# A hand-ordered attention pipeline: scores and kv products a chunk ahead, transposes two ahead, decay split over two engines, dummy products at the start

## What is computed

```
# 1. attention with a decaying state, per head (48 x 48 state)
for t in range(S):
    state = alpha[:, :, t, :, None] * state + einsum('bhd,bhe->bhde', k[t], v[t])
    y[:, :, t] = einsum('bhd,bhde->bhe', q[:, :, t], state)
# 2. Fourier mixing over tokens and width, then a normalised MLP
X = fft(fft(x, axis=1), axis=2);  u = x + real(X)
un = (u - mean(u)) / sqrt(var(u) + 1e-6);  x = u + relu(un @ w_ch1) @ w_ch2
# 3. a token MLP and a channel MLP
u = x + (relu(xT @ w_tok1) @ w_tok2)T;  out = u + relu(u @ w2_ch1) @ w2_ch2
```

## Time and profile before

| what | value |
|---|---|
| median of 3 runs | 998.97 us |
| the profiled execution | 999.33 us, span 997.5 us, mean granted clock 0.991 |
| PE matmuls busy | 926.2 us, 93% of the span |
| DVE, ACT, POOL busy | 473.4, 289.3, 246.7 us |
| chain that ended last | PE 63%, DVE 11%, issue 9%, POOL 6%, ACT 3% |
| stage 0, attention of sequence 0 | 9.07 to 84.5 us, PE busy 65.7 of 75.5 us |
| MLP of sequence 3, alone | 553 to 622 us, PE busy 68.9 of 69 us |
| third layer | 622 to 997 us, PE busy 369.4 of 375 us |

### The profile page before, as it was taken

One profiled execution on the slowest core, in us unless ns is written; L12 is line 12 of the kernel. 1 busy time (PEld: TensorE's weight loads), 2 busy tenths in 40 slices (PEclk: granted clock), 3 DMA queues, 4 the chain that ended last, 5 costly groups with the idle time before them and its releaser, 6 DMA issues.

```text
span 997.5 us, 14828 instructions
## 1 busy us (share of the span) xinstructions
PE 926.2 (93%) x5280; PEld 875.4 (88%) x5280; DVE 473.4 (47%) x1126; ACT 289.3 (29%) x746; POOL 246.7 (25%) x440
## 2 busy tenths in 40 slices
PE   5885689989999989999899999999999999999998
PEld 5774678879888879888799999899999999999998
DVE  5557676554865654865556321622142223313221
ACT  3552243323343332433332322322122112111111
POOL 3677134430244420344401142200020001002000
PEclk9999889999999999999999999999999999999999
DMA  9700402101222003022001600200010001000000
GB/s 280 258 1 1 107 1 54 54 25 44 64 77 56 1 25 107 25 54 55 1 25 46 220 36 1 107 13 24 24 47 0 24 24 47 24 0 24 0 24 24
DMA packets 14235, 50.48 MB, mean 51 GB/s; under 512 B 1392, under 2 KB 5616, under 8 KB 12240
## 3 DMA queue, kind: packets, MB, share of 16 engines
q1 hardware_dynamic: 13600, 46.60, 14.8%
q0 software_dynamic: 576, 3.15, 0.8%
HBM read 40.31 MB, written 9.44 MB: 50 GB/s over the span
## 4 chain that ended last, share of the span: by engine, by line
PE 63%; DVE 11%; issue 9%; POOL 6%; ACT 3%; DMA 0%; DVEq 0%; POOLq 0%; ACTq 0%; SPq 0%
PE bank L1154 20%; PE bank L1156 19%; PE bank L1155 19%; POOL dec L463 3%; DVE ext L714 2%; POOL qkap L447 1%; PE bank L1171 1%; DVE st L729 1%; POOL qkap L444 1%; ACT qz L537 1%; DVE xf L863 1%; DVE at L823 1%; PE bank L1184 1%; DVE tmp L828 1%; DVE hl L1012 1%
## 5 line engine op out<-in xcount | busy, mean ns | idle before, releaser
L1012 DVE SCALAR_TENSOR_TENSOR hl<-bank,hh 128x384 fp32r<-128x384 f32 x192 | 106.1, 552 | 307.6 <-ACT hh L627 307.6
L627 ACT ACTIVATE hh<-bank 128x384 fp32r<-128x384 f32 x192 | 94.0, 490 | 327.9 <-PE bank L1156 327.4
L463 POOL TENSOR_SCALAR dec<-st,suf 48x48 f32<-48x48 f32 x160 | 78.5, 491 | 144.1 <-DVE st L729 88.1
L1154 PE MATMUL bank<-w2h,hh 128*128 128x384 f32 x288 | 102.2, 355 | 5.7 <-DVE u L1027 5.6
L1154 PE MATMUL bank<-nh,w1h 128*128 128x384 f32 x288 | 103.7, 360 | 1.3 <-DVE nl L967 1.3
L537 ACT ACTIVATE qz<-qkap 48x128 f32<-48x128 f32 x192 | 59.2, 308 | 150.9 <-POOL qkap L447 141.2
L1154 PE MATMUL bank<-u2h,w3h 128*128 128x384 f32 x288 | 98.1, 341 | 0.8 <-DVE u2l L1110 0.8
L1156 PE MATMUL bank<-nh,w1l 128*128 128x384 f32 x288 | 98.4, 342 | 0.0
L1155 PE MATMUL bank<-nl,w1h 128*128 128x384 f32 x288 | 98.3, 341 | 0.0
L1154 PE MATMUL bank<-w4h,hh 128*128 128x384 f32 x288 | 97.9, 340 | 0.0
L1156 PE MATMUL bank<-u2h,w3l 128*128 128x384 f32 x288 | 97.5, 339 | 0.0
(11 more groups left out here) (138 smaller groups left out, 1858.2 us busy)
## 6 DMA issues: line engine op xcount, KB each, us to landing
qkap<-qka SPq DMA_DIRECT2D x15, 1008.0 KB, 6.4
vt<-v SPq DMA_DIRECT2D x16, 288.0 KB, 7.7
raw_a<-w_ch SPq DMA_DIRECT2D x6, 768.0 KB, 13.2
mid<-u SPq DMA_DIRECT2D x8, 576.0 KB, 2.7
raw_b<-w_ch SPq DMA_DIRECT2D x6, 768.0 KB, 5.8
xr<-mid SPq DMA_DIRECT2D x8, 576.0 KB, 4.1
out<-u SPq DMA_DIRECT2D x8, 576.0 KB, 2.7
raw_t<-w_tok SPq DMA_DIRECT2D x2, 768.0 KB, 5.1
```

The lines of the kernel that those rows point to most:

```text
L463: pool.tensor_scalar(dec[r, k % 2, e], st[r, (k - 1) % 3, e], suf[r, k % RING, 0:1], None, ALU.mult).then_inc(s_dec, 1)
L627: act.activation(hh[:, s % 4, :], bank[s % 2][:, 0:HALF], ACT.Relu).then_inc(s_hhi, 1)
L1012: dve.scalar_tensor_tensor(out=hl[:, s % 4, :], in0=bank[s % 2][:, 0:HALF], scalar=0.0, in1=hh[:, s % 4, :].bitcast(F32), op0=ALU.max, op1 ...
L1154: pe.matmul(out_ap, wh, rh, start=first, stop=False)
```

## The change

All four pieces of the visit are written anew.

- PE's visit k: scores and now the kv product of chunk k+1 (one semaphore for both), y and state product of chunk k, transpose of chunk k+2. The kv product moves from the y bank into the score bank, the transposed keys into the y bank. In sequences 1 to 3 PE waits at the front for `at` of k and `st` of k; stage 0 alternates two banks of each kind (4, 5 and 6, 7) and waits one visit further back.
- DVE's visit k: `at` of k+1, `st` of k+1 (it was k), scans of k+3. The two reductions of the range test move within the unit; in stage 0 the first unit's reductions read an extra copy of the decays (`alpha0`), and the first suffix product no longer stands behind them.
- POOL's visit k: the two scalings for k+3 first, then one half of `dec` for k+2. The other half is on ACT, at the end of its visit. `dec` gets a third buffer.
- ACT's visit k: `qz` of k+2, `krt` of k+2, `x` of k, its half of `dec` of k+2.
- A visit k = -2 is added in front: `PAUSES` loses slot 1. The scans of chunk 1 leave the Fourier tail of the sequence before and stand in visit -2.
- Stage 0: weight splitting on ACT every second visit from k = 6 (was every visit), on POOL every third from k = 9 (was every second from 10). SP issues queries and keys, then identity and mask, values, the copy of the decays, the other units, and last the flip matrix and column, which have a semaphore of their own. PE starts with 8 products of a zeroed tile, 384 columns each, before its first wait for data.

```diff
-PAUSES = (1, 3, 7, 14, 21, 28)
-VISIT = dict(zip([h for h in range(31) if h not in PAUSES], range(-1, STEPS)))
+PAUSES = (3, 7, 14, 21, 28)
+WARM = 8
+VISIT = dict(zip([h for h in range(31) if h not in PAUSES], range(-2, STEPS)))
...
+    def visit_bank(a, k):
+        return bank[6 + k % 2] if a == 0 else bank[7]
...
# POOL
-            def decay(a, k, lows=0):
...
+            def decay(a, k):
+                if 0 < k < STEPS and k % NC:
+                    pool.wait_ge(s_st, a * STATES + state_index(k - 1) + 1)
+                    pool.tensor_scalar(dec[0:D, k % 3, 0:D], st[0:D, (k - 1) % 3, 0:D], suf[0:D, k % RING, 0:1], None,
+                                       ALU.mult).then_inc(s_dec[0], 1)
+            def visit(a, k):
+                prep(a, k + 3)
+                decay(a, k + 2)
...
# ACT
                 for h in range(2):
                     attn_qz(a, k + 2, h)
-                attn_krt(a, k + 1)
+                attn_krt(a, k + 2)
                 if k >= 0:
                     attn_x(a, k)
+                decay(a, k + 2)
...
# DVE
-                if k >= 0:
-                    attn_state(a, k)
...
+                attn_state(a, k + 1)
+                prep(a, k + 3)
...
# PE
+            def visit(a, k):
...
+                was = k - (1 if a else 2)
+                if 0 <= k + 1 < STEPS:
+                    if was >= -1:
+                        pe.wait_ge(s_at, a * STEPS + was + 2)
+                    if has_state(was + 1):
+                        pe.wait_ge(s_st, a * STATES + state_index(was + 1) + 1)
+                    mm = attn_scores(a, k + 1)
+                    if has_state(k + 1):
+                        mm = attn_kv(a, k + 1)
+                    mm.then_inc(s_sc, 1)
...
+                if k >= 0:
+                    mm = attn_back(a, k)
+                if has_state(k + 2):
+                    mm = attn_turn(a, k + 2)
+                mm.then_inc(s_vis, 1)
...
+            pe.wait_ge(s_zero, 1)
+            for i in range(WARM):
+                pe.matmul(bank[0][:, 0:HALF], at[:, 0, 0, :], at[:, :, :, :].rearrange("p a h t -> p (a h t)")[:, 0:HALF],
+                          start=True, stop=True)
+            pe.wait_ge(s_const, 32)
```

More of the change, by code:

```diff
@@ L542, in attn_x, with decay @@
                     act.wait_ge(s_ua, a * UA)
-                act.wait_ge(s_y, a * STEPS + k + 1)
-                if k % NC < NC - 1:
-                    act.wait_ge(s_st, a * STATES + state_index(k) + 1)
-                act.activation(x[:, k % NC, (k // NC) * PW:(k // NC + 1) * PW], y_bank(a, k)[:, 0:PW], ACT.Copy
-                               ).then_inc(s_x, 1)
+                act.wait_ge(s_vis, visited(a, k))
+                act.activation(x[:, k % NC, (k // NC) * PW:(k // NC + 1) * PW], y_of(a, k), ACT.Copy).then_inc(s_x, 1)
+            def decay(a, k):
+                if 0 < k < STEPS and k % NC:
+                    act.wait_ge(s_st, a * STATES + state_index(k - 1) + 1)
+                    r = head_rows(1)
+                    act.activation(dec[r, k % 3, D:PW], st[r, (k - 1) % 3, D:PW], ACT.Copy, scale=suf[r, k % RING, 0:1]
+                                   ).then_inc(s_dec[1], 1)
             def visit(a, k):
@@ L619, in tail @@
                     norm_split(a, t)
-                if h == SLOTS - 1 and a + 1 < B:
-                    for half in range(2):
-                        attn_qz(a + 1, 0, half)
             def hidden(bi, s):
@@ L1006, in tail @@
                         extreme(a + 1, 0, i)
-                    for k in range(2):
-                        prep(a + 1, k)
+                    prep(a + 1, 0)
             def hidden(bi, s):
@@ L1186, in attn_back @@
                 if c:
-                    pe.wait_ge(s_dec, 2 * s)
-                    mm = pe.matmul(y[:, 0:PW], buf[0:PR, 0, cols], dec[0:PR, k % 2, :], start=False, stop=True)
-                mm.then_inc(s_y, 1)
-                if c < NC - 1:
-                    pe.wait_ge(s_krt, s + 1)
-                    pe.matmul(y[0:PR, KV_AT:KV_AT + PW], krt[:, s % 2, :], vb[:, c, :], start=True, stop=True
-                              ).then_inc(s_kv, 1)
+                    for h in range(2):
+                        pe.wait_ge(s_dec[h], a * STATES + state_index(k - 1) + 1)
+                    mm = pe.matmul(y, buf[0:PR, 0, cols], dec[0:PR, k % 3, :], start=False, stop=True)
+                return mm
+            def visit(a, k):
+                if k == -2 and a:
+                    pe.wait_ge(s_ua, a * UA)
+                    pe.wait_ge(s_nlo, (a - 1) * NC + 2)
+                was = k - (1 if a else 2)
+                if 0 <= k + 1 < STEPS:
+                    if was >= -1:
[6 more added lines that the diff above has]
+                    mm.then_inc(s_sc, 1)
+                if has_state(was + 2):
+                    pe.wait_ge(s_krt, a * STATES + state_index(was + 2) + 1)
+                if was >= 0:
+                    pe.wait_ge(s_x, a * STEPS + was + 1)
+                if k >= 0:
[3 more added lines that the diff above has]
+                mm.then_inc(s_vis, 1)
                 if k == FLAG - 1:
```

244 lines of the change are left out of this document (98 added, 146 removed).

## The result

| | median | runs | profiled execution | span |
|---|---|---|---|---|
| before | 998.97 us | 997.85 to 1000.9 (4) | 999.3 us | 997.5 us |
| after | 939.9 us | 938.46 to 943.73 (4) | 938.46 us | 936.7 us |

The ratio is 0.9413, with a 95% interval of 0.9381 to 0.9445: 59 us less, where 51 were forecast. The mean granted clock is printed as 0.991 before and 0.963 after; the first is too high, for it has 1.00 in stage 0, where score pairs took 1.09 us, against 0.61 at the higher level.

The account below looks back on a forecast made before the run. PE, busy 93% of the span, mostly with MLP matmuls, was taken as the bound. 999.3 - 39.3 (interleaved slots, clock) + 3.9 (sequence starts) - 16 (stage 0) = 947.9, forecast 948 us, own range 940 to 955, whole range 938 to 972.

Parts of the forecast that it names:

- The loop: Interleaved slots: a 3.87 us loop through POOL, ACT and DVE opens; 12.5 of 13.9 us of waits regained a sequence.
- The 1.2 us left for the reductions: Interleaved slots: PE waits of 1.2 us a sequence, expected to remain because of the range reductions on DVE.
- the 0.2 for the sum at slot 29: Interleaved slots: 0.2 us a sequence expected to remain, DVE finishing at 5.65 us and PE coming at 5.45.
- The clock of the second sequence: Second interleaved sequence: the clock's fall behind the stall at slots 27 to 29 goes away, another 1.8 us gained.
- The start of a sequence: First visits of each interleaved sequence: chunk 1's scans move behind the norm statistics; 1.3 us lost each, 3.9 in all.
- Stage 0: Attention ahead of the MLP: earlier scores, clock kept up by dummy products, last result at 68.3 instead of 84.48; gain 16 us.
- The first rival: Stage 0: clock does not stay up, last result at 76, gain 8.5 instead of 16, time 955.5 us; chance 0.25.
- The moved splits: Behind stage 0: POOL's moved weight splits cost nothing; with all seven behind the last result, Fourier start loses 2 us.
- The third layer: Third layer, 375 us: the change was taken to leave it as it is, with no gain.

Follow-up runs that it names:

- Experiment 3: Kernel before, with only the second half of the decayed state moved from POOL to ACT and nothing made earlier: 982.24 us, ratio 0.9832.
- experiment 4: Changed kernel with both halves of `dec` on POOL ahead of its scalings, still two visits ahead, none on ACT: 945.94 us, ratio 0.9468.
- experiment 10: Changed kernel with 128 bytes more of unused room behind the decayed states: 947.3 us, ratio 0.9467.
- experiment 1: Changed kernel without its eight dummy products at the start: 944.55 us, ratio 0.9441.
- experiment 5: Changed kernel with one more product of 384 columns behind each visit of stage 0: 937.24 us, ratio 0.9375.
- experiment 6: Changed kernel with POOL's seven left-over splits held and one more 384-column product behind each visit of stage 0: 927.64 us, ratio 0.9279.
- experiment 9: Changed kernel with 8 splits in the visits, 4 held, and one more 384-column product behind each visit of stage 0: 924.41 us, ratio 0.9243.
- Experiment 2: Changed kernel with POOL's seven left-over weight splits held until DVE has split the folded rows: 936.22 us, ratio 0.9363.
- experiment 7: Kernel before with room for a third decay buffer that nobody uses, moving what lies behind it by 384 bytes: 993.38 us, ratio 0.9933.

## Why the prediction was right, and where its sizes were off

**The loop (right, and sized 1.7 us too small a sequence).** "The `dec` work leaves the loop" and "it now spans two visits" is what the trace shows. "So I take 12.5 of the 13.9 us a sequence as regained": 14.2 came back in the third sequence (87.5 to 73.3), a little more than the 13.9 that were counted as waits. The 1.2 us left for the reductions and the 0.2 for the sum at slot 29 were not lost. Experiment 3 shows that the shortened loop alone would not have done it, experiment 4 that ACT's half adds only 0.65 us. Which of the new distances (decay, transposes, kv product) did it was not separated.

**The clock of the second sequence (right).** It gained 15.1 us where the third gained 13.4; the 1.7 us between them are the 1.8 that were put to the clock behind slot 28, and from 120.4 us on the changed kernel has no fall. The first also gained 15.0, 1.6 more than the third, which no step had. The profile before has PE wait 1.92 us for a normalised row in its first slots, and the one after doesn't; no experiment tested whether that is the whole of it.

**The start of a sequence (right).** 0.9 us lost instead of 1.3, at the three places named.

**Together** the three interleaved stretches gave 43.5 us against 35.4 forecast. These 8.1 us are most of the error.

**Stage 0 (near in time, partly by luck; half right in mechanism).** First scores at 8.38 (9.0 forecast), dummies ending at 8.3 (9.0), last result at 70.18 (68.3). But the forecast rested on the clock staying up, and it did so for about 20 of 60 us only. The first rival's mechanism was at work in the rest, and it put the last result at 76, where stage 0 with the clock low for nearly all of it takes until 73.1 to 73.6 (experiments 10 and 1). The forecast's 68.3 for a kept clock was as much too late: 66.2 to 67.1 in experiments 5, 6 and 9. The distance between the two was right (7.7 us forecast, 6 to 7.4 measured: DVE's, ACT's and POOL's loop takes 2.4 us a visit and PE's slow work 2.69). So the last result came near 68.3 because the clock was up for a third of the stage and both prices were some 2 us too high, and that is luck. The argument against the rival, "no gap would be longer than 1 us, and the falls that I see stand behind near idle stretches", failed: the granted clock went to 0.50 at 18.0 us with PE busy 7.88 of the 11 us around it and no pause longer than 1.2 us before. The trace agrees here with what spoke for the rival (the Trainium skill, "TensorE: Matmul & The Clock Gate", section "A second HAM failure mode: psum-queue depth-cycling"): PE that pauses briefly between groups fell back to half clock and came up again. It doesn't cover the rest of the stage, from 38.5 us on, where PE was busy 29.7 of 30 us and the level stayed low. One product more behind each visit (PE busy 8.6 to 9.2 of 10 us, no pause over 0.8 us) kept it at 1.00.

**The moved splits (the step that failed).** "I cost the moved splits at nothing; with all seven behind the last result the Fourier start would lose 2 us." All seven stood there (the first of them just begun), and it lost 4.3 us. The 2 us took for granted that DVE and POOL go on taking turns as in the earlier trace rows, and they didn't; in experiment 4, where they did beside the same seven splits, the loss was 1.4 us. The Trainium skill ("SBUF — State Buffer", section "SBUF: two separate sides") has the two exclude each other for a whole instruction; the trace agrees with that, and adds that DVE, waiting, was passed over six times running. Experiment 2 shows that the splits are the cause, and that without them the Fourier start would come 6.8 us behind the last result.

**The third layer (not in the prediction).** "The change leaves ... the third layer (375 us) as they are": the instructions yes, the addresses no. 4.1 us of the 4.9 gained behind the last flip are four batches of 1.03 us, and the other 0.8 fit the MLP of the last sequence, whose matmuls mostly take 334 instead of 336 to 339 ns; experiments 7 and 10 switch the batches on and off by the place of the arrays alone.

So the sum in its own terms: interleaved stretches 8.1 us better than forecast, third layer 4.9 better, stage 0 up to the first MLP matmul 3.5 worse (12.5 for 16). That is 9.5 us, against the 9.4 between forecast and profiled execution. The errors partly cancel: experiment 10, which lacks the third layer's gain and whose clock was low for nearly all of stage 0, took 947.3 us, almost the forecast's number, with the same terms off.

## What to carry to other kernels

Where a loop through several in-order engines is longer than the work of the engine that should be full, look for the hand-over that can be made for the visit after next: one of the two `dec` halves on another engine gave 17 us of 999 here, and only the rewrite with hand-overs further ahead made every visit as short as TensorE's own work. A gain ahead of a meeting of DVE and GpSimd must be followed through that meeting: what comes earlier there can meet more of the other engine's work, and two repairs that bring some 3 us each alone can bring 12 together. When a buffer grows, everything behind it moves, and a layer that nobody touched can change by 1%.

## What the runs showed of the hardware

- **DVE behind a row of GpSimd instructions.** Two DVE sums of two SBUF inputs (0.83 us for both, undisturbed) took 11.57, 11.69, 11.58 and 12.85 us beside back-to-back GpSimd splits (1.77 us each) in four kernels, and 2.86 to 3.07 us in four others, in which the engines took turns beside the same splits (2.0 to 2.3 us each then): the kernel before and experiments 3, 4 and 7. Experiment 4 has all seven splits left like the kernels that starved. What decides between turns and starvation was not found.
- **The clock without an idle stretch.** In the changed kernel the granted clock fell to 0.50 at 18.0 us with PE busy 7.9 of the 11 us around it, in short groups with pauses of up to 1.2 us; it fell at 13 us in experiments 2 and 10, behind one such pause. In the kernels with the extra products (busy 8.6 to 9.2 of 10 us, pauses of up to 0.8 us) it stayed at 1.00. From 40 to 70 us PE was busy 29.7 of 30 us with small f32 products and the clock stayed at 0.50 all the same. In the kernel before and in experiment 1 the column prints 1.00 while scores take 1.09 us: durations tell the level, the column doesn't always.
- **Address of the operands.** With weights 128 bytes past a multiple of 256, the third layer ran at 90.07 us a batch with the other operands 128 bytes past one as well, and at 91.1 with these at the multiple (mean 334 against 337 to 339 ns for one product of 384 columns). The last sequence's MLP, alone, shows it too; in the interleaved slots, with the same arrays, the sequence is equally long either way (127.05 and 127.03 us from flip to flip in the changed kernel and in experiment 10). Two kernels of each kind were traced; whether it is the distance to the weights or the address itself that counts wasn't separated.
